# First layer: plain transposes for an expert's rows, its logits computed in four column groups and turned, and a cap on GpSimd's record scatters

## The chip, the cores and the metric

The kernel runs on one core of one Trainium2 chip. The metric is device time in microseconds (us), from the start to the end of one execution. Engines are named as in the profile: PE is TensorE (PEld its weight loads), DVE is VectorE, ACT is ScalarE, POOL is GpSimd, SP is SyncE. All inputs are float32.

## The reference, cut to what matters

Attention with hashed buckets gives x of 1536 tokens by 512 (B is 2 batches). Two expert layers follow.

```python
def moe(x, w_gate, w1, w2):              # first layer: E = 8 experts, F = 1024
    cap = N // E                          # 192 tokens for each expert
    # (token, expert) pairs are taken by falling logit, until an expert has cap tokens
    for e in range(E):
        out[assigned == e] = relu(x[assigned == e] @ w1[e]) @ w2[e]

def moe2(x, w_skip, w_gate, w1, w2):     # second layer
    do = x @ w_skip > 0                   # the other tokens pass through
    logits = x[do] @ w_gate               # 8 logits
    e = argmax(logits); gate = softmax(logits)[e]
    out[do] = x[do] + gate * (relu(x[do] @ w1[e]) @ w2[e])
```

So a token that leaves the first layer needs nine numbers (eight logits and the skip score), each a sum over its 512 features, before the second layer can sort it.

## The kernel before, in words

The kernel has three stages: attention (to about 258 us in the trace), the first expert layer with its assignment (`middle`, to about 522 us), and the second layer (`experts2`). The change is in the first layer and in the sorting for the second one (`regroup`).

**Rounds.** Capacity is assigned in seven rounds, r = 0 to 6. Each round is a chain that passes between DVE and PE: `best` (PE turns each token's best logit into rows, L935), `before` in three parts (DVE compares all tokens with each other and PE counts with L956), `copies` (ACT and DVE move the counts, L1098), `ranks` (PE, L973), `limit` (L978), `taken` (L982), then `places` and `tokens` (L988 and L995), which give the 192 tokens of the expert that has filled up. GpSimd gathers those rows of x (L1280). In each round ACT makes two of the comparison tiles itself, with a Sign and a Relu each (L1092, L1094): steps `sign`.

**Experts.** Work of expert k on its 192 tokens (CAP) is cut into steps: `xt` (two, PE turns the gathered rows, L1006; ACT copies to `xgT`), `h` (eight, first product, L1020; ACT takes two at a time through a Relu to `hT`, L1109), `y` (eight, second product, L1034; ACT copies four at a time to `yT`, L1116), and `rw` (four: `yT` has features on partitions, and it is turned back to rows of tokens). Before the change a `rw` step multiplies two pieces of `yT`, as stationary operand, by `pw2`, whose 137 columns are the identity (128) and that piece's eight gate columns and skip column (L1058). So the same product gives the turned rows and a partial sum of the nine logits. ACT copies the nine columns to `lg4` (L1124) and the rows to `x1` (L1125).

**Order.** `middle_plan` writes one list of steps, and every engine goes through that list in order. Steps of experts wait in the list `work`; between two steps of a round's chain, `fill(n)` takes the next n of them. For rounds from 2 on, the list `some` says how many: 1 between `places` and `best`, 7 between `tokens` and the second `sign`, 2 more ahead of the first `before`, then 4, 3, 1, 1, 1 and 2 ahead of `before` 1, `before` 2, `ranks`, `limit`, `taken` and the next `places`. That is 22 steps in a round. What is left in `work` is appended after the last round, and experts 6 and 7 follow with nothing between their steps but `place`.

**Banks.** The steps share three PSUM banks (`psW`) in rotation. `uses` numbers the uses; `enter` makes PE wait until ACT has emptied use n - 3 (`s_e`). Two `h` steps, or four `y` steps, share one use; an `xt` or an `rw` step has one for itself. As ACT is in order, a copy that stands behind a `sign` step in the list waits for it.

**Sorting for the second layer.** `regroup` works on batches (`place`): tokens of experts 0 to 5 in one batch of 12 half experts, then two, then two. DVE makes records of 12 bytes, and GpSimd scatters them to `rec_d` with one indirect DMA for each half expert (96 tokens, L1489). All but the last two add to one semaphore. SP reads the first 128 records back once 14 scatters have landed (`first_records`, L1574).

SP issues the weight loads of both layers, each after the step that frees its buffer.

Of the kernel before, what the change touches and what calls it, by code (L numbers as in the profile page):

```python
# [5 lines left out]
F32 = mybir.dt.float32  # L6
# [14 lines left out]
P = 128  # L21
# [603 lines left out]

SETS = [[0, 1, 2, 3], [8, 9, 10, 11], [4, 5, 6, 7]]
# [9 lines left out]
def middle_plan():  # L636
# [68 lines left out]
    for k in range(ROUNDS - 1, E):  # L705
        todo = expert(k)

        if k == NEARLY:
            todo.insert(12, ("place", 0, 2 * NEARLY))
        elif k > NEARLY:  # L710
            todo.insert(12, ("place", 2 * k - 2, 2))
# [8 lines left out]
def uses(steps):  # L720

    out = {}
    for s in steps:
        key = {"xt": s, "h": s[:2] + (s[2] // 2,) if s[0] == "h" else s,
               "y": s[:2] + (s[2] // 2,) if s[0] == "y" else s, "rw": s}.get(s[0])
# [16 lines left out]
def middle(nc, io, sb, sem, K, link):  # L742
# [57 lines left out]
    x1 = sb("x1", [HT, NI, DM], F32)  # L800
    lg4 = sb("lg4", [HT, NI, KD, NW], F32)
# [17 lines left out]
    K["s_lg"], K["s_ll"] = sem("logits_copied"), sem("last_logits")  # L819
# [96 lines left out]
    def tensor(pe, place):  # L916
        for st in steps:
# [121 lines left out]
            elif st[0] == "logits":  # L1039
                k, half = E - 1, st[1]  # L1040
                pe.wait_ge(s_e, emptied(("y", k, half)))
                for d in (2 * half, 2 * half + 1):
                    for i in range(2):
                        ins = nc.tensor.matmul(K["psLog"][:, i * NW:(i + 1) * NW], yT[:, k % 2, d, i * HT:(i + 1) * HT],
                                               K["pw2"][:, d, 128:128 + NW], start=d == 0 and i == 0,
# [3 lines left out]
            elif st[0] == "rw":  # L1049
# [4 lines left out]
                if k == 0 and i == 0 and a == 0:  # L1054
                    pe.wait_ge(K["s_const2"], K["n_const2"])
                for c in range(2):
                    d = 2 * a + c
                    ins = nc.tensor.matmul(ps[0:HT, c * 137:c * 137 + 137], yT[:, k % 2, d, i * HT:(i + 1) * HT],  # L1058
                                           K["pw2"][:, d, :], start=True, stop=True)
# [5 lines left out]
    def scalar(act, place):  # L1065
        for st in steps:
# [51 lines left out]
            elif st[0] == "rw":  # L1118
# [3 lines left out]
                v = psW[n % NWB][0:HT, 0:274].rearrange("p (c t) -> p c t", c=2)  # L1122
                if k < E - 1:
                    nc.scalar.copy(lg4[:, 2 * k + i, 2 * a:2 * a + 2, :], v[:, :, 128:137]).then_inc(K["s_lg"], 1)  # L1124
                nc.scalar.copy(x1[:, 2 * k + i, 256 * a:256 * a + 256].rearrange("p (c t) -> p c t", c=2),  # L1125
                               v[:, :, 0:128]).then_inc(s_e, 1)
# [198 lines left out]
def regroup(nc, io, sb, sem, K, link):  # L1325
# [39 lines left out]
    s_ps, s_rs, s_tab, s_th = sem("places"), sem("records_scattered"), sem("tile_table"), sem("passed")  # L1365
# [6 lines left out]
    def vector(dve, i0, n):  # L1372
# [6 lines left out]
        if i0 + n < NI:  # L1379
            dve.wait_ge(K["s_lg"], 2 * (i0 + n))  # L1380
# [102 lines left out]
    def pool(gp, i0, n):  # L1483
# [4 lines left out]
        for i in range(i0, i0 + n):  # L1488
# [496 lines left out]
```

## Time and profile before

| | |
|---|---|
| time, median of 3 runs | 666.3 us (665.94 to 667.8) |
| time of the profiled execution | 669.37 us |
| its span, first to last instruction | 667.6 us |
| mean granted TensorE clock | 0.986 |
| PE busy | 638.4 us (96%) |
| PEld busy | 501.5 us (75%) |
| DVE busy | 361.9 us (54%) |
| ACT busy | 292.0 us (44%) |
| POOL busy | 153.4 us (23%) |

The profiled execution took 3.1 us more than the median of the runs that were only timed. PE's busy time counts modelled ends of overlapping matmuls, so its share says that PE nearly always had something under way, not that it ran at its best rate. A product of float32 operands stands in the trace as two matmul instructions, a transpose as one.

### The profile page before, as it was taken

The numbers are of one execution on the slowest core, as the hardware profiler recorded it, in microseconds if no ns is written. First come the engines' busy times: TensorE is split into PE (matmuls) and PEld (weight loads), VectorE is DVE, ScalarE is ACT, GpSimd is POOL, SyncE is SP. The second block draws the span as 40 slices with busy tenths as digits, with TensorE's granted clock in tenths as the row PEclk, the third lists the DMA queues.
The fourth block names the chain that finished last, engine by engine and source line by source line (L and its number), as shares of the span: only waits on it lengthen the run. The fifth ranks groups of instructions, "written<-read, shape, count | busy, mean of one in ns | idle before, by whom it ended". The sixth has DMA issues, their size and how long they took to land.

```text
span 667.6 us, 11473 instructions
## 1 busy us (share of the span) xinstructions
PE 638.4 (96%) x4400; PEld 501.5 (75%) x4400; DVE 361.9 (54%) x1117; ACT 292.0 (44%) x549; POOL 153.4 (23%) x149
## 2 busy tenths in 40 slices
PE   7999999999999999798999999999959889999996
PEld 4777677677777665387898898989959857767774
DVE  6877767677777768778786867863302220000000
ACT  5867676766776767233352534431111101111110
POOL 5440303132225704101010110102321123322110
PEclk9999999999999999989999999999969989999999
DMA  8975645455563100635372544538973669999940
GB/s 205 232 170 127 160 119 125 118 120 143 160 174 86 32 2 11 236 126 170 109 266 93 194 151 150 181 121 270 375 250 93 225 204 339 355 339 343 354 149 17
DMA packets 73757, 118.45 MB, mean 177 GB/s; under 512 B 33400, under 2 KB 36600, under 8 KB 73426
## 3 DMA queue, kind: packets, MB, share of 16 engines
q1 hardware_dynamic: 69298, 108.72, 53.4%
q0 software_dynamic: 4080, 8.93, 3.8%
q8 instruction: 37, 0.61, 0.4%
q14 instruction: 22, 0.18, 0.1%
q10 hardware_dynamic: 320, 0.01, 0.0%
HBM read 88.13 MB, written 12.36 MB: 151 GB/s over the span
## 4 chain that ended last, share of the span: by engine, by line
PE 86%; DVE 5%; DMA 3%; issue 2%; another core or an unknown queue 2%; ACT 1%; POOL 1%; SPq 0%; POOLq 0%; DVEq 0%
PE psB L1020 13%; PE psB L1034 11%; PE psB L320 9%; PE psB L305 9%; PE psB L1693 9%; PE psB L1679 9%; PE psA L290 6%; PE psA L292 5%; PE psB L1058 2%; PE psB L335 2%; PE psA L956 2%; PE psB L267 2%; PE psB L259 1%; DMA xg<-x_scratch,recs 1%
## 5 line engine op out<-in xcount | busy, mean ns | idle before, releaser
L440 DVE TENSOR_REDUCE mx<-psA 128x1 f32<-128x768 f32 x96 | 91.8, 957 | 45.7 <-PE psA L292 44.1
L508 ACT ACTIVATE prob<-psA,ebi,esc 128x768 f32<-128x768 f32 x96 | 95.8, 998 | 28.8 <-DVE ebi L386 28.8
L1020 PE MATMUL psB<-xgT,w 128*128 128x192 f32 x512 | 94.3, 338 | 0.3 <-ACT xgT L1103 0.3
L1020 PEld LDWEIGHTS psB<-xgT,w 128*128 128x128 f32 x512 | 86.1, 197 | 6.0 <-issue 5.6
L1034 PE MATMUL psB<-hT,w 128*128 128x192 f32 x512 | 88.2, 329 | 0.0
L1034 PEld LDWEIGHTS psB<-hT,w 128*128 128x128 f32 x512 | 82.7, 190 | 0.3
L305 PE MATMUL psB<-cst,prob 128*128 128x128 f32 x576 | 78.7, 273 | 0.3
L290 PE MATMUL psA<-kH,qT 128*128 128x384 f32 x192 | 74.3, 387 | 2.8 <-ACT kB L547 1.6
L559 ACT COPY pT<-psB 128x512 f32<-128x512 f32 x96 | 56.5, 589 | 40.5 <-PE psB L305 39.5
L305 PEld LDWEIGHTS psB<-cst,prob 128*128 128x128 f32 x576 | 67.6, 140 | 6.0 <-DVE pT L453 1.9
L1740 DVE SCALAR_TENSOR_TENSOR ob<-psB,recs,xg 128x512 f32<-128x512 f32 x9 | 6.8, 751 | 117.2 <-PE psB L1693 117.2
L1679 PEld LDWEIGHTS psB<-xgT,w 128*128 128x128 f32 x576 | 65.8, 192 | 5.2 <-issue 5.2
L320 PE MATMUL psB<-pT,v_in 128*64 128x384 f32 x360 | 68.0, 499 | 0.0
L1679 PE MATMUL psB<-xgT,w 128*128 128x128 f32 x576 | 65.8, 275 | 0.8 <-ACT xgT L1723 0.8
L1693 PE MATMUL psB<-w,hT 128*128 128x512 f32 x144 | 66.3, 605 | 0.0
L292 PE MATMUL psA<-kB,qB 128*128 128x384 f32 x192 | 64.8, 338 | 0.0
L290 PEld LDWEIGHTS psA<-kH,qT 128*128 128x128 f32 x192 | 36.1, 188 | 31.7 <-issue 28.7
L1280 POOL DMA_INDIRECT xg<-x_scratch,sidx x16 | 15.4, 961 | 180.9 <-DVE sidx L1168 178.5
L1693 PEld LDWEIGHTS psB<-w,hT 128*128 128x128 f32 x144 | 26.6, 194 | 26.9 <-issue 26.9
L1728 ACT ACTIVATE hT<-psB 128x512 f32<-128x512 f32 x18 | 10.8, 597 | 77.6 <-PE psB L1679 52.1
L582 POOL CAST hi<-raw 128x768 fp32r<-128x768 f32 x16 | 13.6, 852 | 122.5 <-ACT raw L536 107.1
L1109 ACT ACTIVATE hT<-psB 128x384 f32<-128x384 f32 x32 | 15.7, 491 | 58.2 <-PE psB L1020 58.2
(263 smaller groups left out, 886.8 us busy)
## 6 DMA issues: line engine op xcount, KB each, us to landing
w<-in_moe_w SPq DMA_DIRECT2D x34, 2048.0 KB
kH<-hi SPq DMA_DIRECT2D x30, 192.0 KB, 3.5
q_in<-in_q SPq DMA_DIRECT2D x16, 192.0 KB, 3.7
k_in<-in_k SPq DMA_DIRECT2D x16, 192.0 KB, 4.1
v_in<-in_v SPq DMA_DIRECT2D x8, 384.0 KB, 3.4
x_scratch<-x_of_batch SPq DMA_DIRECT2D x2, 1536.0 KB, 7.0
x_scratch<-x SPq DMA_DIRECT2D x8, 384.0 KB, 8.3
qT<-hi SPq DMA_DIRECT2D x15, 192.0 KB, 3.5
```

The costliest lines, as they stand in the source:

```text
L290: nc.tensor.matmul(psS[u % 2][:, half, 0:HALF], qT[:, i, hh, qs], kH[:, i, hh, ks], start=True, stop=False)
L292: ins = nc.tensor.matmul(psS[u % 2][:, half, 0:HALF], qB[:, i, hh, qs], kB[:, i, hh, ks], start=False, stop=True)
L305: ins = nc.tensor.transpose(psT[part][:, at * P:(at + 1) * P], prob[:, u % 2, c // GU, c % GU * P:(c % GU + 1) * P], cst[:, C_ID:C_ID + P])
L320: ins = nc.tensor.matmul(psV[64 * hh:64 * hh + 64, 0:HALF], v_in[:, i, hh, c, :], pT[:, (2 * G + hh) % 4, c, :], start=c == 0, stop=c == N ...
L440: nc.vector.tensor_reduce(mx[:, u:u + 1], psS[u % 2][:, :, 0:HALF], AX.XY, ALU.max).then_inc(s_dv, 1)
L508: nc.scalar.activation(prob[:, u % 2, :, :], psS[u % 2][:, :, 0:HALF], ACT.Exp, bias=ebi[:, u:u + 1], scale=esc[:, u:u + 1], accum_out=den ...
L559: nc.scalar.copy(pT[:, (2 * G + hh) % 4, TD:NC_, c * P:(c + 1) * P], psT[1][:, 0:(NC_ - TD) * P].rearrange("p (c q) -> p c q", c=NC_ - TD) ...
L1020: ins = nc.tensor.matmul(ps[:, (f % 2) * CAP:(f % 2 + 1) * CAP], w1[:, k % 2, d, f * P:(f + 1) * P], xgT[:, k % 2, d, :], start=d == 0, st ...
L1034: ins = nc.tensor.matmul(ps[:, (d % 2) * CAP:(d % 2 + 1) * CAP], w2[:, k % 2, f, d * P:(d + 1) * P], hT[:, k % 2, f, :], start=f == 0, sto ...
L1109: nc.scalar.activation(hT[:, k % 2, f - 1:f + 1, :], psW[n % NWB][:, 0:2 * CAP].rearrange("p (c t) -> p c t", c=2), ACT.Relu).then_inc(s_e, 1)
L1679: ins = nc.tensor.matmul(psH[q][:, f * P:(f + 1) * P], w1[:, k2 % 2, k, (4 * q + f) * P:(4 * q + f + 1) * P], xT[:, t % 2, k, :], start=k ...
L1693: ins = nc.tensor.matmul(psY[t % 2][:, :], hh[:, t % 2, f, :], w2[:, k2 % 2, f, :], start=f == 0, stop=f == KF - 1)
```

## The change

An expert's `rw` step becomes two plain transposes of 128 columns. Two steps are added for experts 0 to 6. `lt` computes the logits from `yT` as moving operand: four products, one for each piece of 128 features, with `pw2` (now 32 columns for each piece, nine of them used) as stationary operand, so that each writes its own 32 partitions of one bank; ACT copies the bank to `lgT`. `lx` turns `lgT` back with two transposes, and ACT copies the nine columns of all four groups to `lg4` at once. `lt` stands after the first two `rw` steps, `lx` after the fourth `h` step. The last expert's logits are computed as before. The list `some` is not touched. The DMAs that brought the identity into `pw2` go, a memset of `pw2` on DVE and a wait of SP for it come. GpSimd keeps three record scatters under way: there are three semaphores, and from the fourth scatter on each waits until the one three before it has landed, except for the last two.

The diff, cut to its core:

```diff
+OPEN = 3
 def expert(k):
-        back = [("rw", k - 1, i, a) for i in range(2) for a in range(2)] if k else []
-        return q + back[:2] + h[:4] + back[2:] + h[4:] + y
+        if k == 0:
+            return q + h + y
+        rw = [("rw", k - 1, i, a) for i in range(2) for a in range(2)]
+        return q + rw[:2] + [("lt", k - 1)] + h[:4] + [("lx", k - 1)] + rw[2:] + h[4:] + y
...
-            todo.insert(12, ("place", 0, 2 * NEARLY))
+            todo.insert(14, ("place", 0, 2 * NEARLY))
...
+    lgT = sb("lgT", [P, CAP], F32)
...
             elif st[0] == "rw":
                 pe.wait_ge(s_e, emptied(("y", k, a)))
                 for c in range(2):
-                    ins = nc.tensor.matmul(ps[0:HT, c * 137:c * 137 + 137], yT[:, k % 2, d, i * HT:(i + 1) * HT],
-                                           K["pw2"][:, d, :], start=True, stop=True)
+                    ins = nc.tensor.transpose(ps[0:HT, c * P:(c + 1) * P], yT[:, k % 2, 2 * a + c, i * HT:(i + 1) * HT],
+                                              cst[:, C_ID:C_ID + P])
+            elif st[0] == "lt":
+                ps = enter(pe, use[st])
+                for d in range(KD):
+                    ins = nc.tensor.matmul(ps[32 * d:32 * d + 32, 0:CAP], K["pw2"][:, d, :], yT[:, k % 2, d, :],
+                                           start=True, stop=True)
+                ins.then_inc(s_f, 1)
+            elif st[0] == "lx":
+                ps = enter(pe, use[st])
+                pe.wait_ge(s_e, emptied(("lt", k)))
+                for i in range(2):
+                    ins = nc.tensor.transpose(ps[0:HT, i * P:(i + 1) * P], lgT[:, i * HT:(i + 1) * HT],
+                                              cst[:, C_ID:C_ID + P])
                 ins.then_inc(s_f, 1)
...
             (ACT, "rw")
-                if k < E - 1:
-                    nc.scalar.copy(lg4[:, 2 * k + i, 2 * a:2 * a + 2, :], v[:, :, 128:137]).then_inc(K["s_lg"], 1)
-                nc.scalar.copy(x1[...].rearrange("p (c t) -> p c t", c=2), v[:, :, 0:128]).then_inc(s_e, 1)
+                nc.scalar.copy(x1[:, 2 * k + i, 256 * a:256 * a + 256], psW[n % NWB][0:HT, 0:256]).then_inc(s_e, 1)
+            elif st[0] == "lt":
+                act.wait_ge(s_f, n + 1)
+                nc.scalar.copy(lgT[:, :], psW[n % NWB][:, 0:CAP]).then_inc(s_e, 1)
+            elif st[0] == "lx":
+                act.wait_ge(s_f, n + 1)
+                nc.scalar.copy(lg4[:, 2 * k:2 * k + 2, :, :], ...).then_inc(s_e, 1)
...
             (regroup, DVE)
-            dve.wait_ge(K["s_lg"], 2 * (i0 + n))
+            dve.wait_ge(K["s_e"], K["use"][("lx", (i0 + n) // 2 - 1)] + 1)
...
             (regroup, POOL)
         for i in range(i0, i0 + n):
+            if OPEN <= i < NI - 2:
+                gp.wait_ge(s_rs[i % OPEN], 16 * (i // OPEN))
             gp.indirect_dma_start(K["rec_d"], ...
-                                  ).then_inc(s_rsl if i0 + n == NI else s_rs, 16)
+                                  ).then_inc(s_rsl if i0 + n == NI else s_rs[i % OPEN], 16)
...
             (SP, first_records)
-        sp.wait_ge(K["s_rs"], 16 * (NI - 2))
+        for n in range(OPEN):
+            sp.wait_ge(K["s_rs"][n], 16 * len(range(n, NI - 2, OPEN)))
...
-        K["pw2"] = sb("pw2", [P, KD, 128 + NW], F32)
+        K["pw2"] = sb("pw2", [P, KD, 32], F32)
...
             (SP)
+            sp.wait_ge(s_c0, 4)
             for k in range(KD):
-                sp.dma_start(K["pw2"][:, k, 0:128], io["consts"][:, C_ID:C_ID + P])
...
             (DVE)
+            nc.vector.memset(K["pw2"][:, :, :], 0.0).then_inc(s_c0, 1)
```

## Rows read from the trace of the kernel before

**Rows 1.** Busy time of each engine in one round (its window, length, engines, clock, DMA)

```profile
402.80:432.00 29.20, 29.20 (x242) 26.39 (x242) 22.54 (x75) 12.59 (x24) 2.03 (x3) 1.00 0.50 173
```

**Rows 2.** Timeline of PE: start, us, engine, line, operation, count

```profile
394.30 0.60 PE L935 MATMUL psB<-cst,m 128*128 128x128 f32 x4
...
466.93 1.10 PE L1058 MATMUL psB<-pw,yT 128*96 128x137 f32 x8
```

**Rows 3.** Chain that ended last: start, us, what (two column groups of 64)

```profile
31.35 1.44 PE psB L320 x8
```

**Rows 4.** Timeline of one round, the chain of DVE, PE and ACT

```profile
383.96 0.62 PE L956 MATMUL psA<-GB,Ob 128*32 128x512 bf16 x8
...
384.84 1.01 ACT L1098 CAST cT<-psA 128x1024 f16<-128x1024 f32 x1 [1.64 <-PE psB L956]
...
386.13 0.45 PE L973 MATMUL psA<-selE,cT 128*128 128x8 f16 x12
...
387.82 0.32 PE L978 MATMUL psA<-cst,cmax 128*128 128x128 f32 x1
...
388.77 0.26 DVE L1250 TENSOR_TENSOR Oa<-Ob,took 128x96 bf16<-128x96 bf16 x1
...
389.28 0.21 PE L982 MATMUL psA<-Oa,onesb 128*128 128x96 bf16 x1
...
391.12 0.18 DVE L1147 TENSOR_TENSOR_SCAN mcum<-onesb,memb 128x12 bf16<-128x12 bf16 x1
...
391.99 0.17 PE L988 MATMUL psA<-memb,strict 128*128 128x12 bf16 x1
...
394.79 0.75 PE L995 MATMUL psA<-tokb,hit 128*128 128x1 f16 x24
...
403.07 0.35 DVE L1227 SCALAR_TENSOR_TENSOR GB<-Rs,m,cst 128x128 bf16<-128x128 f32 x1
```

**Rows 5.** The same timeline, ACT's signs and the first copy behind them

```profile
374.10 1.49 ACT L1092 ACTIVATE Gs<-Rs,m 128x1408 bf16<-128x1408 f32 x1
...
375.63 1.38 ACT L1094 ACTIVATE GA<-Gs 128x1408 bf16<-128x1408 bf16 x1
...
376.96 0.37 ACT L1125 COPY x<-psB 96x256 f32<-96x256 f32 x1
...
397.53 1.36 ACT L1092 ACTIVATE Gs<-Rs,m 128x1280 bf16<-128x1280 f32 x1 [2.39 <-DVE Rs L1189]
...
398.92 1.27 ACT L1094 ACTIVATE GA<-Gs 128x1280 bf16<-128x1280 bf16 x1
```

**Rows 6.** Timeline around the twelve record scatters (the first and the last of them)

```profile
475.19 10.56 PE L1034 MATMUL psB<-hT,w 128*128 128x192 f32 x64
...
475.94 0.97 POOL L1489 DMA_INDIRECT records<-rec,posi  x1 [14.47 <-DVE rec L1419]
...
480.59 0.48 ACT L1116 COPY yT<-psB 128x384 f32<-128x384 f32 x1 [4.71 <-issue]
...
489.50 0.92 POOL L1489 DMA_INDIRECT records<-rec,posi  x1 [0.30 <-issue]
...
493.02 0.48 ACT L1116 COPY yT<-psB 128x384 f32<-128x384 f32 x1 [11.95 <-remote]
...
493.55 2.14 PE L1058 MATMUL psB<-pw,yT 128*96 128x137 f32 x8 [7.14 <-ACT yT L1116]
...
495.48 4.80 PE L1020 MATMUL psB<-xgT,w 128*128 128x192 f32 x18
```

**Rows 7.** Windows of 5 us around a short pause of PE (columns as in rows 1)

```profile
540.00:545.00 5.00, 2.63 (x8) 1.24 (x7) 0.00 (x0) 0.59 (x1) 0.00 (x0) 0.83 0.83 338
545.00:550.00 5.00, 5.00 (x32) 3.84 (x31) 0.75 (x1) 0.00 (x0) 1.07 (x2) 0.83 0.27 57
```

**Rows 8.** DMA issues: count and median us from issue to landing

```profile
records<-rec,posi POOLq DMA_INDIRECT x16, 3.7
```

**Rows 9.** Timeline of DVE at the start: its first work after the memsets

```profile
5.62 1.02 DVE L403 COPY raw<-psA 128x384 f32<-128x384 f32 x2 [3.53 <-PE psA L259]
```

More of the change, by code:

```diff
@@ L708, in middle_plan @@
         if k == NEARLY:
-            todo.insert(12, ("place", 0, 2 * NEARLY))
+            todo.insert(14, ("place", 0, 2 * NEARLY))
         elif k > NEARLY:
-            todo.insert(12, ("place", 2 * k - 2, 2))
+            todo.insert(14, ("place", 2 * k - 2, 2))
         steps += todo
@@ L724, in uses @@
         key = {"xt": s, "h": s[:2] + (s[2] // 2,) if s[0] == "h" else s,
-               "y": s[:2] + (s[2] // 2,) if s[0] == "y" else s, "rw": s}.get(s[0])
+               "y": s[:2] + (s[2] // 2,) if s[0] == "y" else s, "rw": s, "lt": s, "lx": s}.get(s[0])
         if key is not None and key not in out:
@@ L818, in middle @@
     s_w1, s_w2 = K["s_w1"], K["s_w2"]
-    K["s_lg"], K["s_ll"] = sem("logits_copied"), sem("last_logits")
+    K["s_ll"] = sem("last_logits")
     K["psLog"] = psRow[1][0:HT, 0:2 * NW]
@@ L1044, in tensor @@
                         ins = nc.tensor.matmul(K["psLog"][:, i * NW:(i + 1) * NW], yT[:, k % 2, d, i * HT:(i + 1) * HT],
-                                               K["pw2"][:, d, 128:128 + NW], start=d == 0 and i == 0,
+                                               K["pw2"][:, d, 0:NW], start=d == 0 and i == 0,
                                                stop=d == KD - 1, skip_group_check=True)
@@ L1053, in tensor @@
                 pe.wait_ge(s_e, emptied(("y", k, a)))
-                if k == 0 and i == 0 and a == 0:
-                    pe.wait_ge(K["s_const2"], K["n_const2"])
-                for c in range(2):
-                    d = 2 * a + c
-                    ins = nc.tensor.matmul(ps[0:HT, c * 137:c * 137 + 137], yT[:, k % 2, d, i * HT:(i + 1) * HT],
-                                           K["pw2"][:, d, :], start=True, stop=True)
+                for c in range(2):
+                    ins = nc.tensor.transpose(ps[0:HT, c * P:(c + 1) * P], yT[:, k % 2, 2 * a + c, i * HT:(i + 1) * HT],
+                                              cst[:, C_ID:C_ID + P])
+                ins.then_inc(s_f, 1)
+            elif st[0] == "lt":
+                k = st[1]
+                ps = enter(pe, use[st])
+                if k == 0:
+                    pe.wait_ge(K["s_const2"], K["n_const2"])
+                for d in range(KD):
+                    ins = nc.tensor.matmul(ps[32 * d:32 * d + 32, 0:CAP], K["pw2"][:, d, :], yT[:, k % 2, d, :],
+                                           start=True, stop=True)
+                ins.then_inc(s_f, 1)
+            elif st[0] == "lx":
+                k = st[1]
+                ps = enter(pe, use[st])
[3 more added lines that the diff above has]
+                                              cst[:, C_ID:C_ID + P])
                 ins.then_inc(s_f, 1)
@@ L1364, in regroup @@
     s_d, s_e, s_o2, s_pp = sem("logits_shifted"), sem("exp2"), sem("onehot2"), sem("counted2")
-    s_ps, s_rs, s_tab, s_th = sem("places"), sem("records_scattered"), sem("tile_table"), sem("passed")
+    s_ps, s_tab, s_th = sem("places"), sem("tile_table"), sem("passed")
+    s_rs = [sem(f"records_scattered{i}") for i in range(OPEN)]
     s_tot, s_cu, s_sel = sem("totals"), sem("counts_summed"), sem("last_rows_selected")
@@ L1873, in _ @@
                 rows = slice(k * P, (k + 1) * P)
-                sp.dma_start(K["pw2"][:, k, 0:128], io["consts"][:, C_ID:C_ID + P]
+                sp.dma_start(K["pw2"][:, k, 0:E], io["moe2_w_gate"][rows, :]
                              ).then_inc(K["s_const2"], 16)
-                sp.dma_start(K["pw2"][:, k, 128:136], io["moe2_w_gate"][rows, :]
-                             ).then_inc(K["s_const2"], 16)
-                sp.dma_start(K["pw2"][:, k, 136:137], io["moe2_w_skip"][rows].unsqueeze(1)
+                sp.dma_start(K["pw2"][:, k, E:NW], io["moe2_w_skip"][rows].unsqueeze(1)
                              ).then_inc(K["s_const2"], 16)
@@ L1887, in _ @@
                 sp.wait_ge(s_xd[b], 16)
-            sp.wait_ge(K["s_rs"], 16 * (NI - 2))
+            for n in range(OPEN):
+                sp.wait_ge(K["s_rs"][n], 16 * len(range(n, NI - 2, OPEN)))
             sp.wait_ge(K["s_rsl"], 16 * 2)
```

12 lines of the change are left out of this document (8 added, 4 removed).

## The prediction

> **What bounds the kernel now.** I read the busy times of each round first: in a round of 29.20 us PE has something under way for all of it, at full clock, DVE for 22.5 and ACT for 12.6 [rows 1]. The four rounds from 315 us on look alike, so PE sets their length. Then the timeline of one round, to see how close the other bound is: the chain of DVE, ACT and PE that a round consists of. The shortest distance from one PE step of it to the next, with PE always there, is [rows 4]:
> - `places` to `tokens`: 391.99 to 394.79, 2.80 us.
> - `tokens` to `before` 0: 394.79 to DVE's last tile (403.07 + 0.35, and 0.03 to release), 8.66.
> - `before` 2 to `ranks`: 383.96 to the end of ACT's copy (384.84 + 1.01, and 0.06), 1.95.
> - `ranks` to `limit`: 1.69.
> - `limit` to `taken`: 387.82 to 388.77 + 0.26 and 0.06, 1.27 (PE itself came at 389.28).
> - `taken` to `places`: 389.28 to 391.12 + 0.18 and 0.06, 2.08 (PE came at 391.99).
>
> The list `some` fills these gaps well: a step of one `h` (1.3 us) stands in each short one, two `y` steps in the last. So PE hardly ever waits for the chain, and the end of the layer is the sum of PE's work. Last I looked for PE's long waits and found one, at the twelve record scatters, treated below.
>
> **PE's work.** Eight `h` matmuls take 8 x 0.163 = 1.30 us (10.56 us for 64 of them) [rows 6], 1.33 with a change of bank. A `rw` step has four instructions now, (1.10 - 0.28)/7 = 0.117 us apart, so 0.48; a transpose of 128 columns takes (0.60 - 0.27)/3 = 0.11, so the new step takes 0.22 [rows 2]. Saved: 0.26 x 28 steps of experts 0 to 6 = 7.3 us. (The last expert's four stand beside the logits' chain and give nothing.) `lx` is two more transposes, 0.22. `lt` is eight instructions of 192 columns. Four groups of 32 columns with float32 operands are not in the trace; the nearest are two groups of 64, where eight instructions of 384 columns take 1.44 us, that is four pairs 0.32 apart [rows 3]: each pair costs as much as one instruction alone, 384 x 0.163/192. So I take two times 0.163 for the eight, and 0.17 for the change of column groups and back (an estimate: 0.85 for the twelve of a `before` step with its entry, rows 4, less their three times 0.213 as 512 columns of bf16 would take): 0.5 us. Ends: 0.34 without that, and 8 x 0.163 + 0.1 = 1.4 if nothing runs side by side. Added: 7 x 0.72 = 5.0. PE's work falls by 2.3 us.
>
> The pairs start while their predecessor still runs [rows 3], so weight loads are hidden there. [...]
>
> **What the two extra steps do to the order.** This is the largest term. An expert has 24 steps now and a round still takes 22 from the list, so each round from the second on falls two steps further behind, and short steps come to stand in the gaps that an `h` or a `y` used to fill. I wrote out the new list and walked through it with the distances above. Written this way, the same walk gives 29.1 us for each round of the kernel before, with 1 us of waits in all. With the new list PE waits:
> - Round 2: `h` 0 of expert 1 needs the bank of the first `rw` step, and ACT copies that one only behind the second sign, which takes 374.10 to 377.01, 2.9 us, and then 0.37 for the copy [rows 5]. Before, two `h` steps stood between; now `lt` has moved the numbering by one. 2.0 us, and 0.2 ahead of it. `ranks` finds one `rw` (0.22) in place of an `h`: 1.95 - 0.85 - 0.22 = 0.9. Sum 3.1.
> - Round 3: the second sign stands ahead of the copies of `xt`; the second `rw` waits for it: 2.3, and 0.2 at `lt`. `ranks` behind `lx` alone: 0.9. `limit` behind a `rw`: 1.69 - 0.30 - 0.22 = 1.2. `taken` behind a `rw`: 1.27 - 0.16 - 0.22 = 0.9. Sum 5.4.
> - Round 4: the last `h` copy of expert 2 stands behind the first sign (397.53 to 400.19) [rows 5], and `y` needs it: 2.0, and 0.2. `taken` behind `lx`: 0.9. `places` behind two `rw`: 2.08 - 0.04 - 0.44 = 1.6. Sum 4.7.
> - Round 5: `places` 0.5; then `tokens` behind a `rw` and `best`: 2.80 - 0.05 - 0.22 - 1.36 = 1.2. Sum 1.7.
> - Round 6: `ranks` 0.9, `taken` 0.9; behind it `tokens` 6, `places` 7 and `tokens` 7 with 1.2, 0.7 and 1.2, because `lx` and `rw` stand there in place of `y` steps. Sum 4.9.
> - Experts 5 and 6: five short uses of a bank in a row (`xt`, `xt`, `rw`, `rw`, `lt`) ask for banks faster than ACT copies (about 0.4 us each): 0.7 each, 1.5.
>
> Sum 21.3, less the 1 us there now: 20.2. With the work, +17.9 us. Nothing comes back later: whatever a round leaves over is done after the last one, and PE is the bound there too. If the copies behind signs cost nothing it is 6.9 less; if `lt` is serial, 4.6 more.
>
> **The clock.** After a pause of about 2.4 us near 540 (PE busy 2.63 of 5) the granted clock falls, and the mean is 0.83 in two windows of 5 us: 2 x 5 x 0.17 = 1.7 us lost [rows 7]. The list above has five places with 2 us or more of waiting close together. I take two drops' worth, 3.4; the ends are 0 and 5 x 1.7 = 8.5.
>
> **The scatters.** PE's last `y` of expert 6 is done by 485.7, but ACT's copy of it starts at 493.02, and no instruction of the profile releases it ("remote") [rows 6]. PE then waits 7.14 us for that copy. Twelve scatters were issued from 475.94 to 489.50. The release of the first half of the same `y`, with four of them issued, came in time (480.59); the one with eight or more issued came only when the last had landed (489.50 and 3.7) [rows 6, 8]. So I hold that PE's signal got through only once the burst of scatters was over. After the pause PE ran at the lower clock: 2.14 us for eight instructions that take 1.10, and 4.80 for 18 that take 17 x 0.163 + 0.33 = 3.1 [rows 2, 6], 2.7 us more. With three under way the state of four is never passed, so I take 7.1 + 2.7 = 9.8 us off. Ends: nothing, if what counts is the stream and not its depth, and 9.8. The cap itself costs little: three in 3.7 us is one in 1.23, about the present pace (13.56/11 = 1.23) [rows 6, 8]; behind the waiting GpSimd stand only the next batch's scatters, over 15 us later. If landings take 5.6 us under load, the last lands 8 us later, and still ahead of those.
>
> **The rest.** ACT saves four small copies an expert and gets two; it has room [rows 1]. The memset of `pw2` falls where DVE waits 3.53 us at the start [rows 9]; SP's wait is for that, 250 us earlier. Four DMAs of 64 KB go, in a stretch where PE does not wait for SP. Weight loads keep their places relative to the steps that free their buffers. Nothing for all of these.
>
> **Sum.** +17.9 + 3.4 - 9.8 = +11.5 us. On the profiled execution's own 669.4 us that is 680.9; it stands 3.1 over the median, so for the median 666.3 + 11.5 = 677.8. About 2 us (0.3%) is what a measurement of this kernel can tell from no change.
>
> **Rivals.**
> - The scatter wait stays (the stream counts, or the signal is late for another reason): 666.3 + 17.9 + 3.4 = 687.6. For it: no view shows a semaphore of a scatter holding PE's. Chance 0.26. Against it: the release that came in time with four.
> - Faster: the chain gives way. The distances in rows 4 hold because PE's steps come when they do; if DVE and ACT run ahead where fillers are short, the waits largely vanish, and PE's work alone decides: 666.3 - 2.3 - 9.8 = 654.2. It decides if less than 12.1 us of the 20.2 (and of the clock) appear. Against it: ACT and DVE are in order and the rows show their steps back to back. Chance 0.13.
> - Same: the waits cancel the gain of the scatters within 2 us. Chance 0.05.
> [...]
>
> **Chances.** My forecast 0.56, the rivals 0.26, 0.13 and 0.05. Faster 0.13, same 0.05, slower 0.82. The range: forecast's own ends are 666.3 + (17.9 - 6.9) - 9.8 = 667.5 and 666.3 + 17.9 + 4.6 + 5 - 9.8 = 684.0; with the scatter wait 687.6. I give 668 to 688.
>
> **What would show it.** Between 315 and 461 PE's busy time per 29.2 us falls below 29.2; PE waits for ACT's `rw`, `xt` and `hT` copies by about 2 us each, and for DVE at `limit`, `taken`, `places` and `tokens` by about 1 us each; the first `y` of expert 6 starts 17 to 21 us later than 475.19 [rows 6]. No wait of 7 us at the scatters. `lt` takes 0.5 us from its first start to the next step. A PE with no waits in the rounds would prove the walk wrong; a 7 us "remote" wait with three scatters under way would prove the reading of the depth wrong.

## The result, and the profile after

| us | before | changed |
|---|---|---|
| median | 666.7 (665.94 to 667.8, 4 runs) | 676.97 (674.54 to 678.69, 4 runs) |
| profiled execution | 669.37 | 678.69 |
| its span | 667.6 | 676.8 |
| mean granted clock | 0.986 | 0.991 |

The ratio is 1.0149, with a 95% interval of 1.0121 to 1.0177: slower, by 10.3 us in the medians. The forecast was 677.8.

The page's busy times hardly differ from those of before; PE, PEld, DVE, ACT, POOL:

```profile
PE 637.8 (94%) x4406; PEld 494.2 (73%) x4406; DVE 362.6 (54%) x1118; ACT 292.0 (43%) x535; POOL 153.3 (23%) x149
```

PE is busy for 0.6 us less than before in a span that is 9.2 us longer. So what came is hardly work; it is time in which PE has nothing under way. Two windows of one old round's length show where (us, busy time and count of PE, PEld, DVE, ACT, POOL, then clock, DMA share, GB/s); before, the window that begins at 402.80 had PE at 29.20 [rows 1]:

```profile
344.40:373.60 29.20, 23.28 (x194) 19.05 (x192) 18.74 (x66) 12.08 (x20) 2.03 (x3) 0.94 0.40 146
...
402.80:432.00 29.20, 27.67 (x235) 24.08 (x234) 22.59 (x75) 12.32 (x21) 2.03 (x3) 1.00 0.52 172
```

What PE waited for between 300 and 465 us, from the view of waits (us in total, times, longest). In the same stretch PE of the kernel before waited for 1.7 us, in three waits:

```profile
PE psA L994 <- DVE mcum L1177: 2.9, 4, 1.4
PE psA L1001 <- DVE hit L1188: 2.6, 4, 1.0
PE psA L988 <- DVE Oa L1280: 2.4, 3, 0.9
PE psA L979 <- ACT cT L1119: 2.3, 3, 0.8
PE psB L1061 <- ACT xgT L1124: 1.9, 1, 1.9
PE psB L1026 <- ACT x L1143: 1.8, 1, 1.8
PE psA L984 <- DVE cmax L1273: 1.8, 2, 1.0
PE psB L1040 <- ACT hT L1130: 1.7, 1, 1.7
PE psA L941 <- DVE m L1211: 0.3, 1, 0.3
```

Two kinds stand in it. Three waits of 1.7 to 1.9 us, one each, are for a copy of ACT (L1143 is the rows, L1124 `xt`, L1130 `h`). The others, each of 1.4 us or less, are for the next link of the round's chain: `places` (L994), `tokens` (L1001), `taken` (L988), `ranks` (L979), `limit` (L984), `best` (L941). Sum: 17.7 us.

The three long ones in the timeline (start, us, engine, line, operation), each time ACT's sign, the copy behind it, and the PE instruction that waits for the copy:

```profile
315.86 1.38 ACT L1115 ACTIVATE GA<-Gs 128x1408 bf16<-128x1408 bf16 x1
317.15 0.62 ACT L1143 COPY x<-psB 96x256 f32<-96x256 f32 x2
317.55 4.17 PE L1026 MATMUL psB<-xgT,w 128*128 128x192 f32 x24 [1.79 <-ACT x L1143]
...
346.86 1.38 ACT L1115 ACTIVATE GA<-Gs 128x1408 bf16<-128x1408 bf16 x1
348.14 0.84 ACT L1124 COPY xgT<-psB 128x384 f32<-128x384 f32 x2
348.65 0.42 PE L1061 MATMUL psB<-cst,yT 128*96 128x128 f32 x2 [1.94 <-ACT xgT L1124]
...
372.12 1.27 ACT L1115 ACTIVATE GA<-Gs 128x1280 bf16<-128x1280 bf16 x1
373.29 0.47 ACT L1130 ACTIVATE hT<-psB 128x384 f32<-128x384 f32 x1
373.82 8.72 PE L1040 MATMUL psB<-hT,w 128*128 128x192 f32 x52 [1.72 <-ACT hT L1130]
```

In round 3 `ranks` and `limit` come late as well, with one short step ahead of each (L1079 is `lx`, L1061 a `rw`):

```profile
356.61 0.42 PE L1079 MATMUL psB<-cst,lgT 128*96 128x128 f32 x2
...
357.80 0.45 PE L979 MATMUL psA<-selE,cT 128*128 128x8 f16 x12 [0.76 <-ACT cT L1119]
358.11 0.40 PE L1061 MATMUL psB<-cst,yT 128*96 128x128 f32 x2
...
359.50 0.32 PE L984 MATMUL psA<-cst,cmax 128*128 128x128 f32 x1 [0.99 <-DVE cmax L1273]
...
360.83 4.51 PE L1026 MATMUL psB<-xgT,w 128*128 128x192 f32 x16
```

The last row is the clock: 16 such instructions start 16 x 0.163 = 2.6 us after one another at full rate, and here they took 4.5. A window of 5 us around it:

```profile
360.00:365.00 5.00, 4.27 (x17) 4.23 (x17) 3.16 (x15) 0.37 (x1) 0.00 (x0) 0.66 0.24 52
```

The granted clock is 0.66 there, that is 5 x 0.34 = 1.7 us lost; PE was at a granted clock of 0.50 for 3.4 us. In the 5 us before this window it had been busy for 3.25 us.

At the scatters the 7 us wait is gone. GpSimd's first and fourth scatter, ACT's copy of the second half of expert 6's `y`, the `rw` steps that need it, and a later scatter that waited long:

```profile
493.82 0.97 POOL L1523 DMA_INDIRECT records<-rec,posi  x1 [27.26 <-DVE rec L1450]
500.39 0.92 POOL L1523 DMA_INDIRECT records<-rec,posi  x1 [3.12 <-DMA records<-rec,posi]
503.67 0.48 ACT L1137 COPY yT<-psB 128x384 f32<-128x384 f32 x1 [4.72 <-issue]
504.20 0.81 PE L1061 MATMUL psB<-cst,yT 128*96 128x128 f32 x4
...
513.77 0.92 POOL L1523 DMA_INDIRECT records<-rec,posi  x1 [6.29 <-DMA records<-rec,posi]
```

The first of those `y` starts at 493.07, against 475.19 [rows 6]: 17.9 us later. From its start to the `rw` steps it is 504.20 - 493.07 = 11.1 us, against 493.55 - 475.19 = 18.4 [rows 6]: 7.2 less. From its start to the end of the span it is 676.8 - 493.1 = 183.7, against 192.4: 8.7 less. So the profiled executions differ by 17.9 - 8.7 = 9.2 us, and the question is what each of the two numbers is made of.

### The profile page after: what moved, and what is told of

The parts are those of the page before. It is cut to its first block, busy times and chain, and to the rows that moved or that the text cites. A ratio compares the mean times of both kernels' runs of the same rounds, so it can differ in the third digit from the quotient of the medians.

```text
span 676.8 us, 11484 instructions
## 1 busy us (share of the span) xinstructions
PE 637.8 (94%) x4406; PEld 494.2 (73%) x4406; DVE 362.6 (54%) x1118; ACT 292.0 (43%) x535; POOL 153.3 (23%) x149
## 4 chain that ended last, share of the span: by engine, by line
PE 83%; DVE 7%; ACT 3%; DMA 3%; issue 2%; POOL 0%; SPq 0%; DVEq 0%; POOLq 0%; ACTq 0%
PE psB L1026 12%; PE psB L1040 12%; PE psB L320 9%; PE psB L305 9%; PE psB L1728 9%; PE psB L1714 8%; PE psA L290 6%; PE psA L292 5%; PE psB L335 2%; DVE hit L1188 2%; PE psA L962 2%; PE psB L267 2%; PE psB L259 1%; DMA xg<-x_scratch,recs 1%; PE psA L1001 1%
## 5 line engine op out<-in xcount | busy, mean ns | idle before, releaser
L508 ACT ACTIVATE prob<-psA,ebi,esc 128x768 f32<-128x768 f32 x96 | 95.8, 998 | 28.8 <-DVE ebi L386 28.8
L1040 PE MATMUL psB<-hT,w 128*128 128x192 f32 x512 | 86.7, 328 | 1.7 <-ACT hT L1130 1.7
L1130 ACT ACTIVATE hT<-psB 128x384 f32<-128x384 f32 x32 | 15.6, 490 | 66.3 <-PE psB L1026 66.1
L582 POOL CAST hi<-raw 128x768 fp32r<-128x768 f32 x16 | 13.5, 850 | 122.8 <-ACT raw L536 92.5
```

The costliest lines, as they stand in the source:

```text
L508: nc.scalar.activation(prob[:, u % 2, :, :], psS[u % 2][:, :, 0:HALF], ACT.Exp, bias=ebi[:, u:u + 1], scale=esc[:, u:u + 1], accum_out=den ...
L1040: ins = nc.tensor.matmul(ps[:, (d % 2) * CAP:(d % 2 + 1) * CAP], w2[:, k % 2, f, d * P:(d + 1) * P], hT[:, k % 2, f, :], start=f == 0, sto ...
L1130: nc.scalar.activation(hT[:, k % 2, f - 1:f + 1, :], psW[n % NWB][:, 0:2 * CAP].rearrange("p (c t) -> p c t", c=2), ACT.Relu).then_inc(s_e, 1)
```

## Experiments

Each ratio below is against the kernel before, run on the same chip in the same job. The experiments ran in four jobs, each on a chip of its own, and the kernel before does not take the same time in all of them: its median was 666.7 us in the first comparison, then 657.05 (experiments 1 to 4), 657.12 (5 to 8), 656.76 (9 to 11) and 667.65 (12). This turned out to be part of the answer.

### 1. The two new steps are not counted

The first theory is that the list `some` still hands out 22 steps while an expert has 24. Here `fill` hands out `lt` and `lx` in addition.

```diff
     def fill(n):
-        for _ in range(min(n, len(work))):
+        while work and (n > 0 or work[0][0] in ("lt", "lx")):
+            n -= work[0][0] not in ("lt", "lx")
             steps.append(work.pop(0))
```

> The changed kernel, but the list that gives each round its 22 steps does not count lt and lx, so experts stay in step with the rounds. Theory (slipped order plus copies behind signs): the slip and its short gaps go, but one wait for the bank of the first rw step, behind ACT's second sign, is left in every round (about 2 us, five rounds): rounds of 31.0 us, first y of expert 6 at about 485 (before 475.2, changed 493.1), and a median near 667. Rival (the added instructions themselves cost the time): first y of expert 6 stays near 493 and the time near 677.

Measured: 668.6 us (667.3 to 672.97) against 657.05, ratio 1.0183 (1.014 to 1.0225). The order no longer slips: the rounds, `places` to `places`, take 31.3 us and then 30.8 to 30.9 each, and the first `y` of expert 6 starts at 483.1. What is left in them is one wait, the same in every round; it heads PE's waits between 300 and 465 us (all the others together are 1.7, as before the change):

```profile
PE psB L1027 <- ACT x L1144: 9.3, 5, 1.9
```

The round of 380 us, as an example (the sign ends at 380.3, and the copy comes right behind it):

```profile
380.21 0.62 ACT L1144 COPY x<-psB 96x256 f32<-96x256 f32 x2
380.61 4.66 PE L1027 MATMUL psB<-xgT,w 128*128 128x192 f32 x27 [1.85 <-ACT x L1144]
```

So the two links of the argument come apart. The short gaps of the chain are filled again, and their waits are nearly gone. The wait behind the sign stays, because `lt` still takes a bank between the two `rw` steps and the first `h`, and the bank is the one whose copy stands behind the sign. The view counts 1.9 us for it, five times; a round is 1.5 us longer than in experiment 8, which has the same steps without this wait.

This run showed a second thing, in GpSimd's own work. The records of experts 0 to 5 take until 509.7 to go out, and the first gather of the second layer, which must wait for SP to read them back, is late:

```profile
518.71 0.99 POOL L1616 DMA_INDIRECT xg<-x_scratch,recs  x1 [5.68 <-DMA recs<-records]
```

PE waits 3.5 us for its rows (525.6) and runs at half clock (granted 0.50) for 6.8 us there (522 to 529). The cap on scatters has a price that the prediction under-sized. The 11.5 us over the kernel before are then about 5 x 1.5 of the wait in the rounds, and the rest is of the size of this gap and its clock.

### 2. Not counted, and `lt` and `lx` two `h` steps later

```diff
-        return q + rw[:2] + [("lt", k - 1)] + h[:4] + [("lx", k - 1)] + rw[2:] + h[4:] + y
+        return q + rw[:2] + h[:2] + [("lt", k - 1)] + h[2:4] + rw[2:] + h[4:6] + [("lx", k - 1)] + h[6:] + y
```

`fill` is as in experiment 1.

> As e1_uncounted, and lt moved behind two h steps, lx behind the sixth, so that no h step needs a bank whose copy stands behind a sign. Theory: rounds of 29.0 to 29.2 us, no wait over 0.5 us in them, first y of expert 6 at 474 to 476, no long wait at the scatters, median 655 to 658. Rival (added instructions cost the time): near 677. Rival (the scatter wait is not a matter of how many are under way): a 7 us wait is back and the median is near 666.

Measured: 669.6 us (666.41 to 672.39), ratio 1.0186 (1.014 to 1.0231). The rounds take 29.28 to 29.75 us, so the wait behind the sign is gone. But the time did not fall, where 655 to 658 was expected. Moved behind the sixth `h`, `lx` stands right ahead of `place`, which needs its logits, and PE waits 3.57 us at one `place` and 2.33 us at the next:

```profile
473.74 0.32 PE L1497 MATMUL psA<-O,strictb 96*96 96x96 bf16 x1 [3.57 <-DVE O L1424]
```

The first is followed by 6.8 us at half clock (granted 0.50; 16 instructions of `h` took 5.21 us). The edit cured one wait and made two others, which its expectation had not looked for. For the first theory the rounds count, not the total.

### 3. The cap alone, on the kernel before

```diff
+OPEN = 3
...
+            if OPEN <= i < NI - 2:
+                gp.wait_ge(s_rs[i % OPEN], 16 * (i // OPEN))
             gp.indirect_dma_start(K["rec_d"], ...
-                                  ).then_inc(s_rsl if i0 + n == NI else s_rs, 16)
+                                  ).then_inc(s_rsl if i0 + n == NI else s_rs[i % OPEN], 16)
...
```

> The kernel before with nothing but the cap of three record scatters. Theory (with at most three under way PE's release of ACT is not held up): PE's 7.1 us wait at 486 goes, and the time at the lower clock behind it, median 656 to 658. Rival (the wait belongs to the stream of scatters beside the weight loads, whatever its depth): the wait is there, as long or longer, and the median stays 666 to 668.

Measured: 660.16 us (656.42 to 661.95, 10 runs) against 657.05, ratio 1.0045 (1.0016 to 1.0074). No gain; a small loss. The forecast had 9.8 us of gain here. Since the kernel before took 657 on this chip and not 667, the suspicion was that there was no wait here to take away. Experiment 5 looks at that.

### 4. The kernel before with two empty steps an expert

No work is added, none is removed. Only the order slips, as in the change.

```diff
-        return q + back[:2] + h[:4] + back[2:] + h[4:] + y
+        if k == 0:
+            return q + h + y
+        return q + back[:2] + [("none", k - 1, 0)] + h[:4] + [("none", k - 1, 1)] + back[2:] + h[4:] + y
...
-            todo.insert(12, ("place", 0, 2 * NEARLY))
+            todo.insert(14, ("place", 0, 2 * NEARLY))
...
```

> The kernel before with two empty steps for each expert in the places of lt and lx: no engine does anything for them, but they count among the 22 of a round. Theory (the order is what costs): the walk gives round lengths of 27.6, 31.0, 30.6, 28.8 and 30.5 us, first y of expert 6 at about 491 (475.2 + 15.8), the long wait at the scatters as before, and with up to two clock drops a median of 680 to 687. Rival (instructions and copies of lt and lx cost the time): no change, 666.

Measured: 675.54 us (673.62 to 677.39) against 657.05: +18.5 us, ratio 1.0261 (1.0234 to 1.0287). The waits are of the same two kinds, on the old instructions (L1060 is the old `rw`, L975 is `ranks`). The last two rows are the first `y` of expert 6 and ACT's copy of its second half, with all scatters free to go:

```profile
346.23 1.12 PE L1060 MATMUL psB<-pw,yT 128*96 128x137 f32 x4 [1.65 <-ACT xgT L1105]
...
356.65 0.46 PE L975 MATMUL psA<-selE,cT 128*128 128x8 f16 x12 [1.12 <-ACT cT L1100]
...
...
370.98 8.72 PE L1036 MATMUL psB<-hT,w 128*128 128x192 f32 x52 [1.72 <-ACT hT L1111]
...
492.81 10.56 PE L1036 MATMUL psB<-hT,w 128*128 128x192 f32 x64
...
503.41 0.48 ACT L1118 COPY yT<-psB 128x384 f32<-128x384 f32 x1 [4.72 <-PE psB L1036]
```

This is the cleanest of the runs. Two steps that do nothing cost 18.5 us, and the whole change costs 20.6 or, without its cap, 22.0 where the kernel before takes 657 (experiments 6 and 7): what the change adds to the time is, for the most part, its place in the count.

It also tests the walk itself. The rounds from the second on took 28.0, 32.6, 30.6, 29.3 and 32.5 us. The second and the last of these hold a clock drop of 1.7 us each; without them they are 28.0, 30.9, 30.6, 29.3 and 30.8, where the walk gave 27.6, 31.0, 30.6, 28.8 and 30.5. The first `y` of expert 6 starts at 492.8 (expected 491). The expected 680 to 687 held the wait at the scatters, and that is not there: the copy is released at once by PE, with no cap on the scatters.

### 5 and 6. Both kernels again on one chip

Neither kernel is edited; each is run beside the kernel before on a chip where that takes 657.12.

> The kernel before, unchanged, for a profile beside the ones of this job. In the last job it took 657 us where it had taken 666.7, and no experiment there showed the 7 us wait at the scatters. Theory (the wait at the scatters, with the lower clock behind it, is what separates 666.7 from 657): a run near 657 has no PE wait over 2 us at the first transposes of expert 7, a run near 667 has one. Rival (chips differ in something else): the trace is the same as before but for speed everywhere.

> The changed kernel, unchanged, beside the kernel before on this chip. Theory (its 17.9 us in the rounds and two clock drops do not depend on the chip; the scatter wait does): 674 to 680 wherever it runs, so 1.5% over a before that shows the wait and 3.0% over one that does not.

Measured: the kernel before 656.19 us (653.68 to 658.69, 10 runs), ratio 0.999 (0.9968 to 1.0011). The changed one 677.74 us (676.58 to 680.63), ratio 1.0332 (1.0286 to 1.0378). The changed kernel takes the same time as in the first comparison (676.97); it is the kernel before that is 10 us faster here. Its timeline shows why. The first `y` of expert 6, the first and the last of the twelve scatters, a weight load of SP and ACT's copy of the second half of `y` (both wait for the same `y` step of PE), the `rw` steps behind it, and the row selection after the last `place`:

```profile
473.63 10.56 PE L1034 MATMUL psB<-hT,w 128*128 128x192 f32 x64
474.39 0.96 POOL L1489 DMA_INDIRECT records<-rec,posi  x1 [14.47 <-DVE rec L1419]
...
484.23 0.40 SPq L1629 DMA_DIRECT2D w<-in_moe_w  x1
484.23 0.48 ACT L1116 COPY yT<-psB 128x384 f32<-128x384 f32 x1 [4.72 <-PE psB L1034]
484.77 1.18 PE L1058 MATMUL psB<-pw,yT 128*96 128x137 f32 x8
...
487.91 0.92 POOL L1489 DMA_INDIRECT records<-rec,posi  x1 [0.31 <-issue]
...
513.69 2.05 PE L1594 MATMUL psA<-sel,x 96*128 96x128 f32 x16 [0.45 <-DVE sel L1405]
```

The twelve scatters go out just as densely as in rows 6 (13.5 us from the first to the last, 13.56 there), and ACT's copy is released at once by PE. From the start of `y` to `rw` it is 11.1 us, not 18.4, and to the row selection 40.1 us, where it was 49.9 in the first comparison:

```profile
492.00:493.00 1.00, 0.00 (x0) 0.00 (x0) 0.00 (x0) 0.00 (x0) 0.00 (x0) 0.50 0.01 0
493.01 0.40 SPq L1629 DMA_DIRECT2D w<-in_moe_w  x1
...
525.09 2.05 PE L1594 MATMUL psA<-sel,x 96*128 96x128 f32 x16 [0.45 <-DVE sel L1405]
```

The 9.8 us between the two are the wait and the half clock behind it, and they are nearly the whole difference of the medians (666.7 and 656.2). So the same program, with the same twelve scatters issued at the same pace, has the wait in one job and not in another. The rows of the first comparison say two more things. SP's weight load (493.01) and ACT's copy (493.02) wait for the same PE step and went together, so it is PE's signal that was late, and not ACT. And the DMA engines had run empty by then (a share of 0.01 from 492 to 493, the first row): the scatters had landed, but so had the weight load issued at 475.38, and that trace cannot tell which of the two the signal went with.

### 7. The changed kernel without the cap

```diff
-OPEN = 3
+OPEN = 14
```

> The changed kernel with the cap opened to fourteen, so no scatter of the first twelve waits. Theory where before shows no scatter wait: 674 to 680, the cap gave nothing, and the scatters go out 1.23 us apart. Theory where before shows it: 684 to 690. Rival (the cap alone costs time, as it made GpSimd wait 9 us): up to 3 us less than the changed kernel.

Measured, on the chip of experiments 5 and 6: 679.12 us (678.77 to 680.32), ratio 1.0337 (1.0297 to 1.0376); no wait at the scatters. It is the time of experiment 6 within the two intervals. The cap changes nothing that can be measured in the changed kernel where there is no wait to take away. Whether this version has the wait where the kernel before has it was not tried.

### 8. In step, `lt` and `lx` placed well, no cap

`fill` as in experiment 1, `OPEN` as in experiment 7, and

```diff
+        return q + rw[:2] + h[:2] + [("lt", k - 1)] + h[2:4] + [("lx", k - 1)] + rw[2:] + h[4:] + y
```

> The changed kernel in step with the rounds (lt and lx not counted), lt behind two h steps and lx behind four, and no cap. Theory: rounds of 29.0 to 29.3 us, first y of expert 6 at 474 to 476, place no later than before, and the time of the kernel before within 2 us, or 1 us under it, on the same chip (657 or 667). Rival (adding lt and lx costs PE time that the walk leaves out): 5 us or more over before.

Measured: 658.85 us (657.72 to 662.96, 10 runs), ratio 1.0036 (1.0012 to 1.006). Of the 20.6 us that the change costs on this chip, 18.9 are gone against experiment 6. The rounds from the second on take 29.75, 29.28, 29.28, 29.29 and 29.29 us, against 29.20 before: with nothing waiting, they weigh the new work against the old, 0.08 us a round more. An `lt` step and the `h` steps behind it:

```profile
407.61 0.53 PE L1072 MATMUL psB<-yT,pw 128*32 128x192 f32 x8
408.08 2.87 PE L1027 MATMUL psB<-xgT,w 128*128 128x192 f32 x16
```

Where the 2 us that remain over the kernel before come from is less sure. Some 0.5 us is the work above. The rest I looked for at the end of the layer. PE waits 1.15 us for the last `place`, where it was 0.36, and in the profiled execution it then runs at half clock (granted 0.50) for 6.8 us; the row selection behind it, 2.05 us otherwise, took 3.43. The wait:

```profile
514.69 0.21 PE L1497 MATMUL psA<-O,strictb 96*96 96x16 bf16 x1 [1.15 <-DVE O L1424]
```

### 9. The same, with PE kept at work ahead of the last `place`

```diff
             elif st[0] == "place":
+                if st[1] + st[2] == NI:
+                    K["warm"](psRow[0], 5)
```

> e8_in_step_no_cap with five 512-column matmuls on a free bank ahead of the last place step, where PE waits 1.15 us for DVE and the granted clock fell for 6.8 us at 516.9. Theory (a PE with less to do in the tail loses the clock there, which costs 3.4 us): no drop between 505 and 530, 3 us less than e8_in_step_no_cap, so 655 to 656 beside a before of 657, or a little faster than it. Rival (the drop was chance or needs more than this pause filled): 658 to 659 again.

Measured, on another chip than experiment 8 (before: 656.76; expected 655 to 656): 660.51 us (658.67 to 662.25, 12 runs), ratio 1.0042 (1.0022 to 1.0061). The clock did not fall at 517. It fell at 533 instead (0.50 for 6.8 us), during a wait of 3.98 us for the gather of the second layer's next tile:

```profile
534.55 1.11 PE L1704 MATMUL psA<-cst,xg 128*128 128x128 f32 x4 [3.98 <-DMA xg<-x_scratch,recs]
```

In this execution one drop was gone and another one was there; whether the second came because of the first was not tested. The ratio is that of experiment 8. I could not get below the kernel before.

### 10, 11 and 12. The cap again, at six and at three

All three are the kernel before with the edit of experiment 3; experiment 10 has `OPEN = 6`. The first two ran in the job of experiment 9, the last in one of its own.

> The kernel before with a cap of six. Where before takes 657 us: theory (the cap costs through late records: scatters wait for landings beside the weight loads, the first gather moves towards PE's need) gives 656 to 659, between no cap and the 660.2 of three. Where before takes 667: if the number under way decides, the wait at the scatters is 0 to 3 us; if the stream decides, 7 us.

> The kernel before with the cap of three, once more, for a chip where before shows the scatter wait. Where before takes 667: theory (number under way) 657 to 661, rival (stream) 666 to 668. Where before takes 657: 658 to 661 as in e3_cap_alone.

> The kernel before with the cap of three, a last time, in the hope of a chip where the kernel before takes 667 us. There: number under way decides, 657 to 661; the stream decides, 666 to 668. Where before takes 657 nothing new is expected: 658 to 661.

Measured: with six, 657.35 us (10 runs), ratio 0.9983 (0.9957 to 1.001), no difference. With three, 659.46 us (10 runs), ratio 1.0026 (1.0001 to 1.0051), a little slower, as in experiment 3. In the last job the kernel before took 667.65 us (665.23 to 670.11, 7 runs), as in the first comparison, and the cap at three took 658.72 us (658.07 to 660.05): ratio 0.987 (0.9829 to 0.9912), 8.9 us faster. Its timeline (of the kernel with the cap) has the copy in time:

```profile
483.07 0.92 POOL L1494 DMA_INDIRECT records<-rec,posi  x1 [5.52 <-DMA records<-rec,posi]
483.95 0.48 ACT L1118 COPY yT<-psB 128x384 f32<-128x384 f32 x1 [4.72 <-PE psB L1036]
...
508.97 0.99 POOL L1586 DMA_INDIRECT xg<-x_scratch,recs  x1 [4.71 <-DMA recs<-records]
515.08 2.08 PE L1592 MATMUL psA<-cst,xg 128*128 128x128 f32 x8 [3.12 <-DMA xg<-x_scratch,recs]
```

With the cap the kernel takes 658.7 to 660.2 us on all three chips on which it ran; without it 657 or 667. The cap gives 9 us back where the kernel before takes 667, and costs 2.7 to 3.1 us where it takes 657. The rows show that price: a scatter waits for a landing (5.52 us), the first gather is issued at 509.0 and not at 502.8 as in experiment 5, and PE waits 3.1 us for its rows, with a granted clock of 0.50 from 514 to 525. How much of this comes varies: the profiles of experiments 3 and 11 have PE waiting 0.7 and 1.0 us there, at full clock. The kernel before was not profiled in this job; that it had the wait of rows 6 is inferred from its time and from what the cap gave back.

## Why the prediction was right, by its steps

**The time.** 677.8 was forecast and 676.97 measured; the largest term came where it was put. That the number fits so well is luck in part. All four sizes were off: the waits by -4.2 us (16.0 for 20.2), PE's work by +2.8 (0.5 for -2.3), the clock by -1.7 (1.7 for 3.4), the scatters by +1.1 (-8.7 for -9.8). Together they cancel to -2.0, and the profiled execution took 678.7 where 680.9 was forecast for it.

**The order (forecast +20.2 of waits).** The mechanism is shown. Its three long waits are there, at 317.5, 348.7 and 373.8 us, each for the copy named. Round 3's is 2.1 us (348.65 - 346.29, less the 0.22 of the `rw` step between), where 2.3 was forecast; the view of waits counts 1.9, since it counts from modelled ends. The short ones are at the links named. The first `y` of expert 6 starts 17.9 us later, in the range of 17 to 21 that was given. This 17.9 is not the 17.9 of the sum: it holds the clock, and with its clock term the forecast for it was 21.3. Experiment 4 shows that the count does it with no work added (+18.5). The size was too large by about 4: PE's waits of that stretch add up to 17.7, less the 1.7 of before, so 16.0, and the forecast had 20.2. (The walk's terms add up to 21.4, so 20.4; that is rounding.) Of the 4, 1.5 is the last term, the five short uses of a bank in a row: PE shows no wait for a bank between 425 and the `y` of expert 6 (493). Many of the small waits came out 0.1 to 0.3 shorter than their distance less their filler.

**Where the cost shows.** The length of the rounds does not show it. The last `places` is at 460.02, against 455.19 before, only 4.8 us later. The other 13.1 us of the 17.9 come between it and the `y` of expert 6: 1.7 is a clock drop, and the rest are the steps that each round left over. "Whatever a round leaves over is done after the last one" is this; a table of round lengths alone would have found a quarter of the loss.

**PE's work (forecast -2.3).** Wrong in size: it is nothing, or a little more. In experiment 8, with no waits in the rounds, a round is 0.08 us longer than before, 0.5 us for seven experts. `lt` takes 0.47 us from its first start to the next step, and 0.12 ahead of it, together some 0.58 and not 0.5; `lx` takes 0.31 (410.78 to 411.09) and not 0.22. The rest of the shortfall is in the `rw` steps, which save 0.8 us an expert and not 1.03: in a round of experiment 8 the second pair takes 0.48 where it took 1.02, but the first pair 0.85 where it took 1.11. Why the first pair saves only half as much is not shown. The upper end that the prediction gave for `lt`, 1.4 us if nothing runs side by side, did not come: all eight matmuls of an `lt`, in four column groups on the same rows, start within 0.21 us, and the whole step takes 0.58, where eight starts 0.163 apart would take 1.3. The 4.6 us for a serial `lt`, which the forecast's own upper end (684.0) holds, was my estimate and no run shows it: the whole of it would be 7 x (1.4 - 0.5) = 6.3, and how much of that would fall into waits was not shown.

**The clock (forecast +3.4, two drops).** Two drops came in the rounds, at about 361 and 460, each 3.4 us at half rate (granted 0.50), 1.7 lost. But the kernel before had one at about 284 that the changed one did not have, so the net up to the `y` of expert 6 is +1.7. The balance up to there: waits 16.0, work 0.5, clock 1.7, together 18.2, against 17.9 measured; the waits are good to some tenths each. The number of drops is not fixed: up to that `y` the same changed kernel had four in experiment 6 (the first again at 284), and experiment 7, which differs in the cap alone, had two.

**The scatters (forecast -9.8).** The size is right for the first comparison: the wait of 7.2 us is gone and so is the half clock behind it, and 8.7 us came back in all. That the cap did it there is not shown for the changed kernel, since without a cap it ran only where there was no wait. The support is experiment 12, which gives 8.9 for the cap alone on the kernel before. But the reasoning was too simple in one step, that PE's signal got through "only once the burst of scatters was over". Experiment 5 has the same burst, with no wait, and so have the other kernels without a cap, in experiments 4, 7, 8 and 9. A burst of twelve is therefore not enough to hold the signal; something that differs from job to job (the experiments' four jobs each had their own chip) must be added, and what it is stays open. The rows also put the end of the burst earlier than the prediction did (489.50 + 3.7 = 493.2): the DMA engines were empty from 492 on, with the weight load landed too. What can be said is that with three at a time neither the changed kernel nor the kernel before had the wait, in both jobs where the kernel before takes 667. And the cost of the cap was under-sized ("the cap itself costs little"): the pace was worked out from a landing of 3.7 us [rows 8], but in experiment 12 the fourth scatter, which waits for the first (issued at 474.10), went at 483.07, so that a landing took close to 9 us, with the DMA engines at a share of 1.07 from 474 to 484, and 6.6 in the changed kernel (493.82 to 500.39), with a share of 0.92. Without a cap the median over all sixteen was 6.2 in experiment 5, so 3.7 was not a steady price even for the same kernel. The first gather of the second layer waits for the last record. That costs 0.3 to 0.45% (experiments 3 and 11).

**The rivals.** That the scatter wait stays, and that the chain gives way (654.2), are both refuted for the first comparison by its profile. "Same" is refuted by the ratio (1.0121 to 1.0177). There is a case that I had not put among them: no such wait to begin with. Then the change has nothing to gain from its cap: the terms give 657.1 + 17.9 + 3.4 = 678.4, and experiment 6 measured 677.7. So the change costs 1.5% or 3.3%, depending on what the kernel before takes, and ends at the same time in both.

**Still open.** What decides whether PE's release is held while scatters are under way. Whether it depends on how many are open, or on the pace at which they go out beside the weight load, was not told apart: three removes it, twelve has it, and six ran only where there was none.

## What to carry to other kernels

Where a hand-written list fills the gaps of a chain by a count of steps, a new step in the list is priced by what it displaces, not by its own length: here two steps of 0.3 and 0.6 us an expert moved long fillers out of short gaps and copies behind long instructions, and cost some 18 us. Count such steps separately, and look which buffer the next long step waits for and what stands ahead of that buffer's release on its engine. And run the kernel before on more than one chip before a wait without a releaser is made the reason for a change: here the kernel before took 667 us in two jobs of five and 657 in three, and no profile of those three, with all twelve scatters free to go, shows the wait.

## What the runs showed of the hardware

- PE's signal to ACT and to SP came some 7 us late, with no instruction that explains it, around twelve small indirect DMAs and a weight load, in the first comparison; in another job, with the same program and the same pace, it came at once. The kernel took 667 us in two jobs and 657 in three, with all runs of a job within 0.6% of their median.
- The first scatter of a batch (96 records of 12 bytes) took 6.6 us to land in the changed kernel and 9.0 in experiment 12, with the DMA engines at a share of 0.92 and 1.07. The median over all sixteen was 3.7 in one profile of the kernel before [rows 8] and 6.2 in another (experiment 5).
- In an `lt` step, four column groups of 32, all on the same rows, ran side by side with float32 operands: eight instructions of 192 columns started within 0.21 us, where the same width otherwise starts 0.163 us apart (`h`).
- After or during pauses of PE (busy for 3.25 of the 5 us ahead of the window of the drop at 361) the granted clock was 0.50, and 1.00 otherwise, for 3.4 us (at 361 in the changed kernel) or 6.8 us (at 517 in experiment 8) at a time, and for 10.2 us at 488 in the kernel before and at 514 in experiment 12. In experiment 9 the drop at 517 was gone and one at 533 was there.
